# Attention: q and k turned by transposing transfers, sums folded and inverted in small form

## The chip, the cores and the metric

One core of one Trainium2 chip runs the whole program. The metric is the device time of one execution in microseconds (us); the runs of the kernel before lie between 1114.28 and 1118.21, with a median of 1114.59. Beside these runs one execution was taken by the hardware profiler. All rows come from it.

## The reference, cut to what matters

Three layers follow each other. The change is in the first.

```python
def rmsnorm(x, g):                       # q, k: (4, 12, 448, 64)
    return x / np.sqrt(np.mean(x * x, axis=-1, keepdims=True) + 1e-06) * g
q_n, k_n = rmsnorm(q, g_q), rmsnorm(k, g_k)
scores = 1.0 / np.sqrt(64) * np.matmul(q_n, k_n.transpose(0, 1, 3, 2))
attn = np.exp(scores - np.max(scores, axis=-1, keepdims=True))
attn = attn / (np.sum(attn, axis=-1, keepdims=True) + 1e-09)
x = np.matmul(attn, v)                   # rows: 4 * 448, columns: 12 * 64
# second layer: (sigmoid(x @ w_gate) * (x @ w_val)) @ w_out, 768 -> 1536 -> 768
# third layer: one of 8 experts per row, relu(x @ w1[e]) @ w2[e], 768 -> 1024 -> 768
```

## The kernel before

The 48 heads are worked on as 24 pairs (`PAIRS`); a pair is two heads of one batch, whose 64 columns stand side by side in 128. There are no queues worked out by a planner: the program of every engine is an order written by hand, and semaphores (`wait_ge`, `then_inc`) join them. The loop variable `n` of `STEPS` is a step. In step n TensorE computes the scores of pair n, weighs v with the probabilities of pair n-1 and computes the leading scores of pair n+1, from which the row maxima come.

The way of one pair through the engines:

- SP (SyncE) issues the load of q and k (`load_qk`, L457) as 112 rows with 4 x 64 x 2 numbers each for q and for k, and the loads of v (`load_v`, L463 and L468). It waits on nothing else in this part.
- ScalarE squares the rows (`take_squares`, L736), VectorE sums them per head (`mean_squares`, L979), GpSimd raises the means to the power -1/2 (`inverse_rms`, L566 and L569) and scales the rows of q and k in place (`normalise`, L578).
- TensorE turns the scaled rows by eight 112x128 transposes in f32 (`turn_qk`, L1389) into PSUM. ScalarE copies them as f16 (`high_qk`, L758 for q with the gain of both norms and L759 for k), VectorE writes what the f16 rounding left (`low_q` L1006, `low_k` L1013). Both halves are in `qk_t`, a ring of three.
- TensorE multiplies the high halves (`leading`, L1406, in four blocks j of 112 rows), VectorE takes the negated maxima (`maxima`, L1019), TensorE turns these (`turn_max`, L1413) and VectorE spreads them over the blocks (`shift_rows`, L1026).
- `scores(n, i)` (L1429, L1431), i from 0 to 3, are the full products in three f16 passes with the shift added. i = 0 holds the last 64 keys, the others 128 keys each. All four go to the same two banks of PSUM, so `scores(n, i+1)` waits for `exps(n, i)` on ScalarE (L765 for i = 0, L767 else).
- The probabilities of the last 64 keys are split in f16 halves (`end_high` L773 on ScalarE, `end_low` L606 on GpSimd), as is v (`v_high` L778, `v_low` L1033); TensorE weighs them in `weigh_end` (L1443). The 384 other keys are weighed in f32 (`weigh`, L1452), for each of the two heads h in three chunks; each product is two instructions. v stands beside a block of constants there, so the same product gives the row sums, 64 times the same.
- ScalarE copies the sums and the result to SBUF (`take_out(n, h)`, L785 and L786). VectorE inverts all 128x448 sums (`invert_sums`, L1039), GpSimd multiplies (`weigh_out`, L585), ScalarE and GpSimd split the result in two f16 halves (`x_high` L790, `x_low` L589) for the next layer.

What sets the order around the change: `weigh_end(n-1)` waits for `take_out(n-2, 1)`, because both use the same banks. `turn_qk` shares its banks with `leading`. ScalarE's program for one step is `take_out(n-2,1)`, `exps(n,0)`, squares, `end_high`, `exps(n,1)`, `take_out(n-1,0)`, `exps(n,2)`, `x_high`, `high_qk(n+2)`, `v_high`, `exps(n,3)`. Near the end it also splits the first weights of the second layer (`split_up`, L710, and `turned_high`, L716); on VectorE the corresponding part and the routing weights (L955, L967) wait for the last x. The first layer-two product (L1543) needs only the x of the first batch. L736 is also the line of the squares at the start, and L720 of the load of the constants, whose first 128 columns are the identity for the transposes. L1375 is filler work on TensorE at the start.

Of the kernel before, what the change touches and what calls it, by code (L numbers as in the profile page):

```python
# [18 lines left out]
S_OP = 256.0  # L19
# [38 lines left out]
def attention_moe_moe_kernel(nc, qk, v, v_last, g_qk, w_gate, w_val, w_out, w_out_t, router_w, out_gate_w,  # L58
# [14 lines left out]
    KCH = KEYS // 128  # L73
    assert S - KEYS == 64 == D
# [3 lines left out]
    with ctx:  # L78
# [55 lines left out]
        qk_t = [at.take(128, 4 * S, F16).rearrange("p (x l s) -> p x l s", x=2, l=2) for _ in range(3)]  # L134
# [6 lines left out]
        x_raw = [at2.take(128, S, F32) for _ in range(2)]  # L141
        sums = [at2.take(128, S, F32) for _ in range(2)]
# [113 lines left out]

        y_dram = nc.dram_tensor("y_parts", [N, 2 * DM], F16).ap()
# [3 lines left out]

        const_loaded = sem("const_loaded")
# [36 lines left out]
        sums_inv_ready = sem("sums_inv_ready")  # L299
# [141 lines left out]
        STEPS = range(PAIRS + 2)  # L441
# [4 lines left out]
        def _(sp):  # L446
# [7 lines left out]
            def load_qk(n):  # L454

                wait(sp, qk_turned, n - 3)
                sp.dma_start(qk_raw[n % 4].rearrange("p x j c -> p x (j c)"), qk_d[n]).then_inc(qk_loaded[n % 4], 16)  # L457
# [13 lines left out]
            load_qk(1)  # L471
            for n in range(2, 4):
                load_qk(n)
            for n in range(3):
                load_v(n)
            for n in range(4, PAIRS + 5):
                if 3 <= n - 5:
                    load_v(n - 5)
                if has(n):
                    load_qk(n)  # L480
# [80 lines left out]
        def _(pool):  # L561
            def inverse_rms(n):
# [3 lines left out]
                nc.gpsimd.tensor_scalar(rms_sq, mean_sq[n % 2], 1e-6, 1.0, ALU.add, ALU.mult).then_inc(rms_ready, 1)  # L566
                pool.wait_ge(rms_ready, n + 1)
# [3 lines left out]
            def normalise(n):  # L571

                pool.wait_ge(rms_inv_ready, n + 1)
                xs = slice(0, 1) if n == 0 else slice(0, 2)
# [6 lines left out]
            def weigh_out(n):  # L581

                pool.wait_ge(sums_inv_ready, n + 1)
                pool.wait_ge(o_taken, 4 * n + 4)
                nc.gpsimd.tensor_tensor(x_out[n % 2], x_raw[n % 2], sums_inv[n % 2], ALU.mult).then_inc(x_ready, 1)  # L585
# [24 lines left out]
            for n in STEPS:  # L610
# [3 lines left out]
                if has(n - 2):  # L614
                    weigh_out(n - 2)
                if has(n):
                    end_low(n)
                if has(n - 2):
                    x_low(n - 2)
# [85 lines left out]
        def _(act):  # L705
# [13 lines left out]
            act.dma_start(gains, g_qk).then_inc(gains_loaded, 16)  # L719
            act.dma_start(cst, consts).then_inc(const_loaded, 16)  # L720
# [39 lines left out]

            def exps(n, i):
# [18 lines left out]
            def take_out(n, h):  # L780

                act.wait_ge(o_ready, 2 * n + h + 1)
                wait(act, x_ready, n - 1)
                o_rows, sum_rows = slice(h * D, (h + 1) * D), slice((1 - h) * D, (2 - h) * D)
                nc.scalar.activation(sums[n % 2][o_rows], ps[sum_rows, 6 + h, SQ], ACT.Copy, bias=1e-9 * S_OP).then_inc(o_taken, 1)  # L785
                nc.scalar.activation(x_raw[n % 2][o_rows], ps[o_rows, 6 + h, SQ], ACT.Copy).then_inc(o_taken, 1)  # L786
# [19 lines left out]
            for n in STEPS:  # L806
                if n == 1:
                    load_up_weights()
                if n == 2:
                    load_router()  # L810
                if n == PAIRS - 3:
                    split_up(0, 0)
# [6 lines left out]
                if has(n + 4) and n > 0:  # L819
                    take_squares(n + 4 if n > 1 else 4)  # L820
                if has(n):
                    end_high(n)
                    exps(n, 1)
                if has(n - 1):
                    take_out(n - 1, 0)
                if has(n):
                    exps(n, 2)
                if n == 0:
                    exps(n, 3)
                if n == 1:  # L830
                    take_squares(5)
                if has(n - 2):
                    x_high(n - 2)
                if has(n + 2):
                    high_qk(n + 2)
                if has(n):
                    v_high(n)
                if has(n) and n > 0:
                    exps(n, 3)
# [102 lines left out]
        def _(dve):  # L942
# [93 lines left out]
            def invert_sums(n):  # L1036
                dve.wait_ge(o_taken, 4 * n + 3)
                wait(dve, x_ready, n - 1)
                nc.vector.reciprocal(sums_inv[n % 2], sums[n % 2]).then_inc(sums_inv_ready, 1)  # L1039
# [7 lines left out]
            dve.wait_ge(const_loaded, 16)  # L1047
# [10 lines left out]
            low_k(0)  # L1058
            shift_rows(0)
# [3 lines left out]
            for n in STEPS:  # L1063
                if has(n - 1):
                    v_low(n - 1)
                if has(n - 2):
                    invert_sums(n - 2)
                if has(n + 1):
                    maxima(n + 1, 0)
                    maxima(n + 1, 1)  # L1070
                if n == 1:
                    mean_squares(4)
                if has(n + 1):
                    maxima(n + 1, 2)
                    maxima(n + 1, 3)
                if has(n + 4) and n > 0:
                    mean_squares(n + 4)
                if has(n + 1):
                    shift_rows(n + 1)
                if has(n + 2):  # L1080
                    low_q(n + 2)
                    low_k(n + 2)
# [286 lines left out]
        def _(pe):  # L1369
# [24 lines left out]
            def leading(n, j):  # L1394

                if j == 0:
# [37 lines left out]
            def weigh_end(n):  # L1434

                pe.wait_ge(v_lo_ready, n + 1)
                pe.wait_ge(p_lo_ready, n + 1)
# [31 lines left out]
            pe.wait_ge(const_loaded, 16)  # L1469
# [24 lines left out]
            for n in STEPS[1:]:  # L1494
                if has(n):
                    scores(n, 0)
                if has(n + 1) and n > 1:
                    leading(n + 1, 0)
                if n == PAIRS:
# [229 lines left out]
```

## Time and profile before

| | |
|---|---|
| median of 3 runs | 1114.59 us |
| profiled execution: time / span | 1117.86 us / 1116.1 us |
| granted clock of TensorE, mean | 0.996 |
| busy over the span: TensorE products, VectorE, ScalarE, GpSimd | 98%, 53%, 38%, 22% |
| attention part, from the start to the first product of the second layer | 295.48 us |

The busy share is a mean over very different stages: in the attention part all engines are well used, in the later layers TensorE works nearly alone. So the attention part has to be read by itself, by stretches and by its timeline. The time of the profiled execution is 1.76 us longer than its span; the rows count from the span's start.

### The profile page before, as it was taken

The page shows a single profiled execution, that of the slowest core. Times are in us where ns is not written, and L with a number is a line of the kernel's source. Part 1 is how long each engine was busy: PE and PEld are TensorE (multiplying, and loading weights), DVE is VectorE, ACT ScalarE, POOL GpSimd, SP SyncE. Part 2 cuts the span into 40 slices and gives each one's busy share as a digit, 9 for nine tenths or more (in the row PEclk, how much of TensorE's full clock was granted, in tenths as well). Part 3 has the DMA queues.
Part 4 walks back from the last instruction along what each step waited for, and adds up shares of the span by engine and source line. Part 5 has one row for each costly group of instructions (what it writes and reads, how often), then busy time and mean ns, then how long its engine had stood idle before and what let it go on. Part 6 is the DMA issues. An engine that isn't in the chain of part 4 may idle for free.

```text
span 1116.1 us, 17825 instructions
## 1 busy us (share of the span) xinstructions
PE 1092.4 (98%) x6616; PEld 571.7 (51%) x6617; DVE 594.7 (53%) x840; ACT 428.6 (38%) x632; POOL 250.0 (22%) x237
## 2 busy tenths in 40 slices
PE   7999999999999999999999999999999999999997
PEld 3444444443455555555555555556455555555554
DVE  6889888887633333333343331104565555556841
ACT  5777787777511111111111220001343443443531
POOL 4767676772200000000000100000111112111211
PEclk9999999999999999999999999999999999999999
DMA  5522121200121111111100332100375455456710
GB/s 137 135 52 73 51 74 51 71 22 18 43 86 57 58 56 56 56 56 56 56 29 1 119 136 70 43 28 29 138 252 190 156 185 204 142 194 225 270 36 18
DMA packets 72026, 104.11 MB, mean 93 GB/s; under 512 B 29344, under 2 KB 47918, under 8 KB 71968
## 3 DMA queue, kind: packets, MB, share of 16 engines
q1 hardware_dynamic: 63536, 89.84, 24.7%
q0 software_dynamic: 3168, 11.02, 2.9%
q10 hardware_dynamic: 5264, 2.49, 0.9%
q8 instruction: 36, 0.59, 0.2%
q14 instruction: 22, 0.18, 0.1%
HBM read 93.88 MB, written 13.76 MB: 96 GB/s over the span
## 4 chain that ended last, share of the span: by engine, by line
PE 93%; DMA 2%; ACT 2%; DVE 1%; issue 1%; ACTq 0%; POOL 0%; POOLq 0%; DVEq 0%; SPq 0%
PE ps L1543 29%; PE ps L1558 14%; PE ps L1615 12%; PE ps L1637 12%; PE ps L1452 10%; PE ps L1429 5%; PE ps L1406 2%; PE ps L1389 2%; PE ps L1443 2%; PE ps L1431 1%; PE ps L1624 1%; PE ps L1602 1%; DMA arena<-y_parts,arena 1%; DMA arena<-in_constants 1%; PE ps L1684 1%
## 5 line engine op out<-in xcount | busy, mean ns | idle before, releaser
L1543 PE MATMUL ps<-arena 128*128 128x448 f16 x1728 | 328.8, 352 | 0.0
L1543 PEld LDWEIGHTS ps<-arena 128*128 128x128 f16 x1728 | 168.2, 98 | 156.1 <-issue 0.5
L1558 PE MATMUL ps<-arena 128*128 128x392 f16 (+1 forms) x996 | 165.3, 329 | 0.0
L1615 PE MATMUL ps<-arena 128*128 128x512 f16 x648 | 147.3, 382 | 1.2 <-DVE arena L1322 1.2
L1123 DVE SCALAR_TENSOR_TENSOR arena<-arena 128x768 f16<-128x768 f32 (+1 forms) x112 | 112.8, 1068 | 65.3 <-ACT arena L878 64.5
L1637 PE MATMUL ps<-arena 128*128 128x384 f16 x816 | 135.4, 326 | 0.0
L1452 PE MATMUL ps<-arena 128*128 128x448 f32 x288 | 132.2, 569 | 0.0
L1558 PEld LDWEIGHTS ps<-arena 128*128 (+1 forms) x996 | 97.3, 98 | 66.9
L845 ACT ACTIVATE arena<-ps 128x448 f32<-128x448 f32 x48 | 26.1, 544 | 262.7 <-PE ps L1543 262.6
L1097 DVE SCALAR_TENSOR_TENSOR arena<-ps,arena 128x448 f32<-128x448 f32 x48 | 30.0, 625 | 175.6 <-PE ps L1543 95.7
L878 ACT ACTIVATE arena<-arena 128x768 f16<-128x768 f32 (+1 forms) x112 | 99.3, 928 | 41.6 <-DMA arena<-in_moe_w 37.4
L1019 DVE TENSOR_REDUCE arena<-ps 112x2 f16<-112x896 f32 x96 | 99.0, 1077 | 17.1 <-PE ps L1406 17.1
L1637 PEld LDWEIGHTS ps<-arena 128*128 128x128 f16 x816 | 79.1, 98 | 50.6
L1615 PEld LDWEIGHTS ps<-arena 128*128 128x128 f16 x648 | 62.9, 98 | 73.1 <-issue 2.4
L767 ACT ACTIVATE arena<-ps,arena 128x896 f32<-128x896 f32 x72 | 72.5, 1008 | 27.7 <-PE ps L1431 27.6
L1039 DVE RECIPROCAL arena<-arena 128x448 f32<-128x448 f32 x24 | 70.9, 2953 | 10.4 <-ACT arena L785 10.4
L660 POOL MEMSET arena<- 128x1536 f16 x1 | 1.4, 1378 | 323.8 <-PE ps L1543 323.8
L1429 PE MATMUL ps<-arena 64*128 64x448 f16 (+1 forms) x576 | 71.1, 352 | 1.9 <-DVE arena L1026 0.7
L1452 PEld LDWEIGHTS ps<-arena 128*128 128x128 f32 x288 | 47.4, 190 | 45.3 <-issue 45.3
L1157 DVE TENSOR_SCALAR arena<-ps 128x16 f32 (+1 forms) x12 | 2.1, 175 | 112.4 <-ACT arena L862 112.4
L569 POOL TENSOR_TENSOR arena<-arena 112x16 f32<-112x16 f32 x21 | 60.9, 2901 | 1.8
L862 ACT ACTIVATE arena<-ps 128x768 f16<-128x768 f32 x13 | 10.5, 811 | 126.3 <-PE ps L1558 126.3
(181 smaller groups left out, 1045.5 us busy)
## 6 DMA issues: line engine op xcount, KB each, us to landing
arena<-in_moe_w SPq DMA_DIRECT2D x48, 512.0 KB, 4.8
arena<-in_moe_w SPq DMA_DIRECT2D x64, 384.0 KB, 4.7
arena<-in_qk SPq DMA_DIRECT2D x23, 448.0 KB, 3.6
y_parts<-arena SPq DMA_DIRECT2D x16, 384.0 KB, 2.3
arena<-in_v SPq DMA_DIRECT2D x48, 96.0 KB, 2.5
arena<-in_moe_w_out SPq DMA_DIRECT2D x12, 384.0 KB, 5.3
arena<-in_w_out_t SPq DMA_DIRECT2D x11, 384.0 KB, 3.1
arena<-in_moe_w_gate SPq DMA_DIRECT2D x10, 384.0 KB, 4.2
```

Of the source, the lines that this page charges most:

```text
L569: nc.gpsimd.tensor_tensor(rms_inv, rms_sq, minus_half, ALU.pow).then_inc(rms_inv_ready, 1)
L767: nc.scalar.activation(probs[n % 2][:, :, i - 1], ps_pair(score_slot(n, i), 128), ACT.Exp, bias=lift[:, 1:2])\
L878: nc.scalar.activation(hi, raw_rows(e, p), ACT.Copy, scale=S_OP).then_inc(w_hi_ready, 1)
L1019: nc.vector.tensor_reduce(neg_max[n % 2][:, :, j], ps_pair(max_slot(n, j)), AX_X, ALU.max, negate=True)\
L1039: nc.vector.reciprocal(sums_inv[n % 2], sums[n % 2]).then_inc(sums_inv_ready, 1)
L1123: nc.vector.scalar_tensor_tensor(lo, raw_rows(e, p), S_OP, hi, ALU.mult, ALU.subtract).then_inc(w_lo_ready, 1)
L1429: nc.tensor.matmul(outs[h], qk_t[n % 3][rows, 1, kl, ks], qk_t[n % 3][rows, 0, ql], start=(kl + ql == 0), stop=False)
L1452: last = nc.tensor.matmul(ps[:, 6 + h, SQ], v_ones[n % 3][:, c, h * D:h * D + 2 * D], probs[n % 2][:, h, c], start=False, stop=(c == KCH - 1))
L1543: last = nc.tensor.matmul(ps[:, 2 * (b % 2) + g, 0:S], up_w[s][:, g, c, wl], xt[:, b * KC + c, xl], start=(c == 0 and wl + xl == 0), stop= ...
L1558: last = nc.tensor.matmul(ps[:, 4 + 2 * s + h, 0:cols], gt[:, f, gl, bass.ds(t * 128, 128)], wo[:, f, wl, h, 0:cols], start=(f == 0 and gl ...
L1615: last = nc.tensor.matmul(ps[:, b, :], x_t[:, xl, c], w1_s[s][:, c, wl, b * 512:(b + 1) * 512], start=(c == 0 and xl + wl == 0), stop=(c = ...
L1637: last = nc.tensor.matmul(ps[:, 4 + h, 0:HALF_DM], hid_t[:, b, hl, c], w2_s[s][k][:, wl, h * HALF_DM:(h + 1) * HALF_DM], start=(k == 0 and ...
```

## The change

1. From pair 5 on (`TURNED = 5`, the sixth) TensorE does not turn q and k. GpSimd multiplies the rows of q by both gains (`gain_rows`, prepared once by VectorE from a new input `g_rows`) before it scales; ScalarE writes the f16 copy of the rows (`rows_high`), VectorE the rest (`rows_low`), and SP issues two transposing transfers, one for each f16 half, from the rows to `qk_t`, whose layout is changed for it. `leading(n, 0)` waits for them.
2. The sums are not inverted 128x448 wide. SP moves one row of each head's sums into 64 partitions of 7 (`move_sums`), VectorE inverts 128x7, SP saves the result in HBM, waits for this, and loads it spread over 64 partitions again (`spread_inverse`). `weigh_out`, `x_high` and `x_low` come one step later, so `STEPS` has one more; `x_raw` and `sums` have three buffers.
3. `end_low` goes from GpSimd to VectorE from the fourth pair on, and from step 3 on the orders of TensorE, ScalarE and VectorE are written anew. Steps 0 to 2 keep the old order nearly.
4. The constants are loaded in two pieces, the identity first (`eye_loaded`); the gains' load goes from ScalarE's queue to SP's.

```diff
-        STEPS = range(PAIRS + 2)
+        STEPS = range(PAIRS + 3)
...
+            def move_sums(n):
+                sp.wait_ge(o_taken, 4 * n + 3)
+                wait(sp, few_inv_ready, n - 1)
+                for h in range(2):
+                    sp.dma_start(few_sums[n % 2][h * D:(h + 1) * D],
+                                 sums[n % 3][h * D:h * D + 1].rearrange("o (p c) -> o p c", c=S // D)).then_inc(sums_moved[n % 2], 16)
+            def move_rows(n):
+                sp.wait_ge(rows_lo_ready, n - TURNED + 1)
+                sp.wait_ge(scores_ready, 4 * (n - 2))
+                for l in range(2):
+                    sp.dma_start_transpose(qk_t_blocks[n % 3][:, l], rows_parts[n % 2][:, l]).then_inc(qk_moved[n % 3], 16)
+            def spread_inverse(n):
+                sp.wait_ge(few_inv_ready, n + 1)
+                wait(sp, x_ready, n - 1)
+                sp.dma_start(inv_dram[n % 2].rearrange("h (p c) -> (h p) c", c=S // D), few_inv[n % 2]).then_inc(inv_saved[n % 2], 16)
+                sp.wait_ge(inv_saved[n % 2], 16 * (n // 2) + 16)
+                for h in range(2):
+                    sp.dma_start(sums_inv[n % 2][h * D:(h + 1) * D], inv_dram[n % 2, h].unsqueeze(0).to_broadcast([D, S]))\
+                        .then_inc(inv_spread[n % 2], 16)
+            for n in range(2, PAIRS + 2):
+                move_sums(n - 2)
+                if has(n + 1):
+                    load_v(n + 1)
+                if n + 2 >= TURNED and has(n + 2):
+                    move_rows(n + 2)
+                if has(n + 6):
+                    load_qk(n + 6)
+                spread_inverse(n - 2)
...  GpSimd, in inverse_rms(n)
+                if n >= TURNED:
+                    pool.wait_ge(gain_rows_ready, 1)
+                    nc.gpsimd.tensor_tensor(qk_raw[n % 4][:, 0], qk_raw[n % 4][:, 0], gain_rows.unsqueeze(1).to_broadcast([PT, J, 2 * D]),
+                                            ALU.mult).then_inc(q_gained, 1)
...  GpSimd, loop of the steps: x one step later
-                if has(n - 2):
-                    weigh_out(n - 2)
-                if has(n):
+                if has(n - 3):
+                    weigh_out(n - 3)
+                    x_low(n - 3)
+                if n < 3:
                     end_low(n)
...  ScalarE
-            act.dma_start(gains, g_qk).then_inc(gains_loaded, 16)
-            act.dma_start(cst, consts).then_inc(const_loaded, 16)
+            act.dma_start(cst[:, 0:128], consts[:, 0:128]).then_inc(eye_loaded, 16)
+            act.dma_start(cst[:, 128:CONST_COLS], consts[:, 128:CONST_COLS]).then_inc(const_loaded, 16)
...
+            def rows_high(n):
+                act.wait_ge(qk_normed, n + 1)
+                if n - 2 >= TURNED:
+                    act.wait_ge(qk_moved[(n - 2) % 3], moved(n - 2))
+                nc.scalar.activation(rows_parts[n % 2][:, 0], qk_raw[n % 4].rearrange("p x j c -> p (x j c)"), ACT.Copy)\
+                    .then_inc(rows_hi_ready, 1)
...  ScalarE's steps from 3 on
                     take_out(n - 2, 1)
                     exps(n, 0)
+                    end_high(n)
+                    v_high(n)
+                    exps(n, 1)
+                    take_squares(n + 4)
+                    exps(n, 2)
+                x_high(n - 3)
                     take_out(n - 1, 0)
                     exps(n, 3)
+                    rows_high(n + 3)
...  VectorE
             def invert_sums(n):
-                nc.vector.reciprocal(sums_inv[n % 2], sums[n % 2]).then_inc(sums_inv_ready, 1)
+                dve.wait_ge(sums_moved[n % 2], 32 * (n // 2) + 32)
+                nc.vector.reciprocal(few_inv[n % 2], few_sums[n % 2]).then_inc(few_inv_ready, 1)
...  VectorE's steps from 3 on: rows_low(n+2), maxima(n+1,0), v_low(n), maxima(n+1,1), end_low(n),
...  invert_sums(n-2), maxima(n+1,2), mean_squares(n+4), maxima(n+1,3), shift_rows(n+1)
...  TensorE's steps from 3 on
                     scores(n, 0)
                     leading(n + 1, 0)
+                    leading(n + 1, 1)
                     weigh_end(n - 1)
-                    weigh(n - 1, 0, (0,))
-                    leading(n + 1, 1)
                     scores(n, 1)
-                    weigh(n - 1, 0, (1, 2))
+                    weigh(n - 1, 0, (0,))
                     leading(n + 1, 2)
-                    leading(n + 1, 3)
+                    weigh(n - 1, 0, (1,))
                     scores(n, 2)
+                    weigh(n - 1, 0, (2,))
+                    leading(n + 1, 3)
                     weigh(n - 1, 1, (0,))
-                    turn_qk(n + 2)
                     scores(n, 3)
                     turn_max(n + 1)
                     weigh(n - 1, 1, (1, 2))
```

## Rows read from the trace of the kernel before

**Rows 1.** Busy time of each engine in one stretch of the attention part.

```profile
core 0: us, PE busy (x) PEld busy (x) DVE busy (x) ACT busy (x) POOL busy (x), PEclk, DMA share, GB/s
...
140.00:160.00 20.00, 19.84 (x118) 8.25 (x116) 17.69 (x18) 15.42 (x25) 15.36 (x12) 1.00 0.25 70
```

**Rows 2.** TensorE's timeline over one step: start, duration, line.

```profile
153.01 0.76 PE L1429 MATMUL ps<-arena 64*64 64x448 f16 x6
...
153.88 0.40 PE L1406 MATMUL ps<-arena 64*112 64x448 f16 x2
154.36 0.74 PE L1443 MATMUL ps<-arena 64*128 64x448 f16 x6
155.03 1.02 PE L1452 MATMUL ps<-arena 128*128 128x448 f32 x2
155.98 0.40 PE L1406 MATMUL ps<-arena 64*112 64x448 f16 x2
156.22 0.73 PE L1429 MATMUL ps<-arena 64*128 64x448 f16 x6
...
157.06 1.77 PE L1452 MATMUL ps<-arena 128*128 128x448 f32 x4
158.77 0.59 PE L1406 MATMUL ps<-arena 64*112 64x448 f16 x4
...
160.04 1.02 PE L1452 MATMUL ps<-arena 128*128 128x448 f32 x2
...
161.76 0.74 PE L1429 MATMUL ps<-arena 64*128 64x448 f16 x6
...
164.34 0.76 PE L1429 MATMUL ps<-arena 64*64 64x448 f16 x6
```

**Rows 3.** ScalarE's timeline in the same step.

```profile
153.12 0.54 ACT L785 ACTIVATE arena<-ps 64x448 f32<-64x448 f32 x1 [0.42 <-PE ps L1452]
...
154.77 1.05 ACT L736 ACTIVATE arena<-arena 112x1024 f32<-112x1024 f32 x1
155.72 0.57 ACT L773 ACTIVATE arena<-arena 128x448 f16<-128x448 f32 x1
157.18 1.01 ACT L767 ACTIVATE arena<-ps,arena 128x896 f32<-128x896 f32 x1 [0.89 <-PE ps L1431]
```

**Rows 4.** VectorE's groups by shape, first 345 us: count | busy us, mean ns.

```profile
L1039 DVE RECIPROCAL arena<-arena 128x448 f32<-128x448 f32 x24 | 70.9, 2953 | 10.4 <-ACT arena L785 10.4
...
L1103 DVE TENSOR_TENSOR arena<-arena 128x448 f16<-128x448 f32 x7 | 4.4, 626 | 0.2
```

**Rows 5.** Timeline of the start, ScalarE's queue and three engines.

```profile
1.27 0.45 ACTq L719 DMA_DIRECT2D arena<-in_g_qk  x1
...
7.00 1.47 POOL L578 TENSOR_TENSOR arena<-arena 112x512 f32<-112x512 f32 x1 [4.69 <-DVE arena L993]
...
9.81 1.06 ACT L736 ACTIVATE arena<-arena 112x1024 f32<-112x1024 f32 x1 [1.95 <-DMA arena<-in_qk]
...
10.46 1.13 PE L1389 MATMUL ps<-arena 112*128 112x112 f32 x8 [3.27 <-DMA arena<-in_constants]
```

**Rows 6.** The SP queue's issues in one step, with their time.

```profile
139.19 0.32 SPq L457 DMA_DIRECT2D arena<-in_qk  x1
141.78 1.24 SPq L463 DMA_DIRECT2D arena<-in_v  x2
```

**Rows 7.** DMA from 100 to 200 us: size of one, us to landing.

```profile
arena<-in_qk SPq DMA_DIRECT2D x9, 448.0 KB, 3.5
...
arena<-in_v_last SPq DMA_DIRECT2D x17, 16.0 KB, 2.4
```

**Rows 8.** DMA of the first 12 us, the gains' load.

```profile
arena<-in_g_qk ACTq DMA_DIRECT2D x1, 1.0 KB, 5.8
```

**Rows 9.** Timeline of the last steps and the hand-over.

```profile
257.32 0.74 PE L1443 MATMUL ps<-arena 64*128 64x448 f16 x6 [1.06 <-ACT arena L786]
...
302.00 0.19 DVE L967 TENSOR_SCALAR arena<-ps 128x32 f32<-128x32 f32 x1 [2.96 <-POOL arena L589]
```

**Rows 10.** The chain that ended last, start and length.

```profile
295.48 23.84 PE ps L1543 x126
```

More of the change, by code:

```diff
@@ L73, in attention_moe_moe_kernel @@
     KCH = KEYS // 128
+    TURNED = 5
     assert S - KEYS == 64 == D
@@ L805, in _ @@
             high_qk(1)
-            for n in STEPS:
+            for n in range(3):
                 if n == 1:
@@ L810, in _ @@
                     load_router()
+                    take_out(0, 1)
+                exps(n, 0)
+                if n > 0:
+                    take_squares(n + 4 if n > 1 else 4)
+                end_high(n)
+                exps(n, 1)
+                if n > 0:
+                    take_out(n - 1, 0)
+                exps(n, 2)
+                if n == 0:
+                    exps(n, 3)
+                if n == 1:
+                    take_squares(5)
+                high_qk(n + 2)
+                v_high(n)
+                if n > 0:
+                    exps(n, 3)
+            rows_high(TURNED)
+            for n in STEPS[3:]:
                 if n == PAIRS - 3:
@@ L826, in _ @@
                 if has(n):
-                    exps(n, 2)
-                if n == 0:
                     exps(n, 3)
[L830 to L839, printed above, removed]
+                if has(n + 3):
+                    rows_high(n + 3)
             def chunk(f, s):
@@ L1062, in _ @@
             mean_squares(3)
-            for n in STEPS:
-                if has(n - 1):
+            for n in range(3):
+                if n > 0:
                     v_low(n - 1)
+                maxima(n + 1, 0)
+                maxima(n + 1, 1)
+                if n == 1:
+                    mean_squares(4)
+                if n == 2:
+                    dve.wait_ge(gain_rows_loaded, 16)
+                    nc.vector.scalar_tensor_tensor(gain_rows, gain_raw[:, 0:2 * D], float(D) ** -0.5, gain_raw[:, 2 * D:4 * D],
+                                                   ALU.mult, ALU.mult).then_inc(gain_rows_ready, 1)
+                    invert_sums(0)
+                maxima(n + 1, 2)
+                maxima(n + 1, 3)
+                if n > 0:
+                    mean_squares(n + 4)
+                shift_rows(n + 1)
+                low_q(n + 2)
+                low_k(n + 2)
+            v_low(2)
+            for n in STEPS[3:]:
+                if has(n + 2):
+                    rows_low(n + 2)
+                if has(n + 1):
+                    maxima(n + 1, 0)
+                if has(n):
+                    v_low(n)
+                if has(n + 1):
+                    maxima(n + 1, 1)
+                if has(n):
+                    end_low(n)
                 if has(n - 2):
@@ L1068, in _ @@
                 if has(n + 1):
[L1069 to L1073, printed above, removed]
                     maxima(n + 1, 2)
[L1075 to L1076 removed]
+                if has(n + 4):
                     mean_squares(n + 4)
                 if has(n + 1):
+                    maxima(n + 1, 3)
                     shift_rows(n + 1)
[L1080 to L1082 removed]
                 if n == PAIRS - 2:
@@ L1493, in _ @@
             turn_max(1)
-            for n in STEPS[1:]:
+            for n in range(1, 3):
+                scores(n, 0)
+                if n > 1:
+                    leading(n + 1, 0)
+                weigh_end(n - 1)
+                weigh(n - 1, 0, (0,))
+                if n == 1:
+                    leading(n + 1, 0)
+                leading(n + 1, 1)
+                scores(n, 1)
+                weigh(n - 1, 0, (1, 2))
+                leading(n + 1, 2)
+                leading(n + 1, 3)
+                scores(n, 2)
+                weigh(n - 1, 1, (0,))
+                turn_qk(n + 2)
+                scores(n, 3)
+                turn_max(n + 1)
+                weigh(n - 1, 1, (1, 2))
+            for n in STEPS[3:]:
                 if has(n):
                     scores(n, 0)
-                if has(n + 1) and n > 1:
+                if has(n + 1):
                     leading(n + 1, 0)
+                    leading(n + 1, 1)
                 if n == PAIRS:
```

106 lines of the change are left out of this document (73 added, 33 removed).

## The prediction

> **What bounds the kernel now.** I read the table of stretches first. In a stretch in the middle of the attention part TensorE is busy 19.84 of 20 us at full granted clock; VectorE is next with 17.69, then ScalarE with 15.42 and GpSimd with 15.36 [rows 1]. So here TensorE is the bound. Its timeline then gives the period: pair by pair the same order repeats, from the first `scores` product at 153.01 to the next at 164.34, 11.33 us [rows 2]. The reader should take the starts, not the busy times, because matmuls overlap. The chain of waits says the same thing. From the moment TensorE starts on the next layer the change touches nothing. What moves the time is therefore the attention stage: start, 24 steps, hand-over.
>
> **Steady steps (3 to 20, 18 of them).** Removed: the eight `turn_qk` transposes. Two f32 products of `weigh`, the turn behind them and the start of `scores` take 160.04 to 161.76, 1.72; two such products with an f16 product right behind take 155.03 to 155.98, 0.95 [rows 2]. The turn is worth 0.77 us.
>
> Moved: `leading(n+1,1)` now stands ahead of `weigh_end`. In the old order TensorE has one `leading` between `scores` and `weigh_end`, starting at 153.88, and `weigh_end` starts 0.48 later; one `leading` elsewhere needs 0.24 (155.98 to 156.22) [rows 2]. The missing 0.24 is a wait: `weigh_end` needs both copies of `take_out`, which ScalarE began at 153.12, and starts 1.24 after that [rows 2, 3]. The second `leading` fills exactly this hole: 0.24 saved.
>
> Added: the f32 products of `weigh` stand in five groups, not four. Four products at once take 1.71 (157.06 to 158.77), two take 0.95, so the split costs 2 x 0.95 - 1.71 = 0.19 [rows 2]. TensorE alone: 11.33 - 0.77 - 0.24 + 0.19 = 10.51.
>
> ScalarE now has `rows_high` between the last exponentials and `take_out`. The square of 112x1024, 1.05 long, starts 0.95 before its successor [rows 3], so I take 0.95 for the copy of the same shape and 0.91 for exponentials of 1.01 by the same overlap. The last `scores` starts 2.58 before the next step [rows 2]; exponentials start 0.96 after their `scores` (157.18 against 156.22) [rows 2, 3]. So they start at -1.62, `rows_high` at -0.71, `take_out` at +0.24 instead of +0.11. `weigh_end` may then start at 0.24 + 1.24 = 1.48, and TensorE is there at 0.87 + 2 x 0.24 = 1.35. A wait of 0.13 remains: 10.64 a step. Saving 18 x 0.69 = 12.4. Bounds: 14.8 if there is no such wait; 7.9 if `rows_high` and the exponentials cost their full durations and the wait is 0.38.
>
> The other engines: VectorE has 17.69 of 20, which is 10.0 a step [rows 1]. It loses the 2.95 us reciprocal, gains `rows_low` (no row of this shape; at least the 0.63 of a 448-wide subtraction, at most 1024/448 of it, 1.43; I take 1.4) and `end_low` at 0.63 [rows 4]. That is 9.1 with `low_q` and `low_k` still counted, below 10.64. The small reciprocal is 1/64 as wide; I cost it at 0.2. GpSimd has 8.7, gains the q gain (the 512-wide multiplication took 1.47 [rows 5]) and loses a subtraction of about 1.0: 9.2, hidden by the 10.64 of TensorE. ScalarE has 8.7, gains 0.95, loses the two copies of `high_qk`: hidden except for the 0.13 above. If this cover were gone, VectorE or GpSimd would have to be 1.5 us slower a step to count.
>
> **The SP queue** is the dangerous term, because everything there is in one row and blocks. A step issues: two `move_sums`, four loads of v, two transposing transfers, one load of q and k, one save, a wait for that save, two spreads. Issue times: 1.24 for two loads of v, so 0.62 each, which I take for every transfer of short pieces, and 0.32 for the load with long rows [rows 6]. `move_sums` 1.24, v 2.50, qk 0.32, save to landing 2.4 like the 16 KB load [rows 7], spreads 0.64 to 1.24: 7.1 to 7.7, I take 7.4. With T for one transposing issue the queue's loop is 7.4 + 2T. It stays hidden under 10.64 up to T = 1.62. No row shows T. Nearest from below 0.32, from above 0.62 [rows 6]; if each of a transfer's eight 112x128 blocks cost such an issue, T would be 8 x 0.62 = 5.0. I take a value between 0.6 and 1.6, nearest to the rows of one issue, and cost it at nothing, hidden by TensorE's step. The transfers carry 229 KB each; the 448 KB load lands in 3.5 [rows 7], so both together should land in about 4. They are issued at about 4.6 into the step (`take_out`'s first copy at 0.8, `move_sums` and v 3.74) and are needed at 0.87 of the next: 6.9 us of room. The Trainium skill, in "DMA: Bandwidth & Descriptors", section "Latency and other measured facts", gives 261 GB/s for a DMA transpose; an estimate from it is 458 KB / 261 GB/s = 1.8 us for both, and the sum would stay as it is. No row of this trace shows a transposing transfer, so nothing here confirms it.
>
> The sums' way is hidden: folded sums are wanted by VectorE after `end_low`, about 5.2 into the step, and land at 0.8 + 0.6 + 2.4 = 3.8. If they were late by more than 1.4, the third and fourth `maxima` and then `turn_max` would be next.
>
> **Start.** TensorE's first turn begins at 10.46, released by the constants' DMA [rows 5]. It needs only the identity, now a load of its own in the place of the gains' one, which was issued at 1.27 and landed 5.8 later, at 7.1 [rows 5, 8]. The scaled q was ready at 7.00 + 1.47 = 8.47, so at most 1.9 is gained. But ScalarE squares pair 2 at 9.81, for 1.06, ahead of the first `high_qk` [rows 5], which can pull the gain to 0.9 or, if the loads land otherwise, to 0. I take -1.5.
>
> **Entry into step 3.** GpSimd's gain for pair 5 waits for VectorE's `gain_rows`, which stands behind two maxima in step 2; the scaling and `rows_high(5)` follow, and `take_out` stands behind that. I take +0.5, from 0 to 1.5.
>
> **Steps 21 to 23.** In step 21 `weigh_end` waited 1.06 for ScalarE's split of weights [rows 9]; that split stays, so nearly nothing comes back. Step 22 loses its wait and gets the order's gain, 0.6; step 23 merges its weigh groups, 0.5. Together -1.2.
>
> **Hand-over.** VectorE got the last x at 302.00 after a wait of 2.96 on GpSimd, 6.5 after TensorE began the next layer at 295.48 [rows 9, 10]. Now three transfers of about 2.4 replace the 2.95 reciprocal [rows 4, 7]: some 5 later, 11.5 to 12 after that start. TensorE waits for the first gate result only after four sums of 18 products, and 126 products take 23.84 there [rows 10], so after 13.6. Up to 2 us of cover, of which ScalarE's gate itself takes about half. I take +0.5, from 0 to 3.
>
> **Sum:** -12.4 - 1.5 + 0.5 - 1.2 + 0.5 = -14.1. The profiled execution took 1117.86 (span 1116.1, 1.8 around it), so it becomes 1103.8; it lies 3.3 above the median of 1114.59. On the median: 1100.5.
>
> **Rivals.** (a) As forecast, 1097 to 1105: 0.50.
> (b) The SP queue sets the step mildly, T between 1.62 and 1.9, or ScalarE's wait is the full 0.38: the step is 10.9 to 11.2 and the time 1105 to 1111. For it speaks that the queue is within 1.6 us of the step at T = 0.8; against it that an ordinary issue takes 0.32 to 0.62. 0.20.
> (c) Slower: the transposing issue holds SP for T over 2.0. From there the loop, 7.4 + 2T, passes 11.33 by more than start and end give back. At T = 2.5 it is 12.4, 19 x 1.07 = +20, less the 1.7 of start and end: 1133. For it: a wait for a landing and a dozen issues share one queue which before was idle most of a step; save and spreads stand behind 458 KB and the next 448 KB load. 0.22 with (d).
> (d) The transfers run block by block, each block its own fixed cost. With the row of 0.62 per block, 16 blocks are 9.9 and the loop is 17.3: 19 x 6.0 = +114, 1226. This part of (c) has 0.07. A page of the Trainium skill, "VectorE: DVE Perf Modes", section "The three transpose paths", speaks this way: 1309 ns for one 128x128 by DMA against 390 by TensorE. Taken block after block its figure would be an estimate of 21 us a pair; nothing in this trace bears it out.
> (e) No change: gains and a slightly long queue cancel, T near 1.96, 1109 to 1120: 0.08.
>
> A measurement of this kernel can tell about 0.5%, 5.6 us, from no change. Faster by more: (a) and most of (b), 0.65. Within: the rest of (b) and (e), 0.12. Slower: 0.23. The range runs from 1097 (no ScalarE wait and the full start: -14.8 - 1.9 - 1.2) to 1128, T = 2.4; (d) and the upper part of (c), about 0.15, are left out. The likeliest case alone has 1097 to 1105.
>
> **What would show it.** Right: the period from `scores(n,0)` to the next at 10.6 to 10.8; `leading(n+1,0)` released by TensorE's own order, not by a DMA; SP idle at the top of `move_sums`; `weigh_end` waiting about 0.1 on `take_out`; TensorE's first turn at about 8.6. Wrong: `leading` with a wait on a DMA, transposing issues over 1.7 us, SP's wait for `o_taken` gone, VectorE waiting for the sums.

## The result

The changed kernel took 1126.94 us (median, 1124.74 to 1127.79) against 1116.07 for the kernel before (four runs each): ratio 1.0096, 95% interval 1.008 to 1.0113. It is slower by about 11 us, where 14 less were forecast. It lies inside the stated range, among the slower outcomes, to which 0.23 was given.

The stretch of the attention part that answers to [rows 1], with its columns in the same order (TensorE, its weight loads, VectorE, ScalarE, GpSimd):

```profile
140.00:160.00 20.00, 17.07 (x96) 6.08 (x94) 14.85 (x17) 14.83 (x22) 14.85 (x11) 1.00 0.51 126
```

No engine is near 20 of 20 (TensorE has 17.07), at full granted clock. No engine that computes is the bound. TensorE's timeline over one step, against [rows 2]:

```profile
146.24 0.76 PE L1551 MATMUL ps<-arena 64*64 64x448 f16 x6
...
154.34 0.74 PE L1551 MATMUL ps<-arena 64*128 64x448 f16 x6
154.92 0.35 PE L1553 MATMUL ps<-arena 64*128 64x448 f16 x2
156.41 0.22 PE L1535 MATMUL ps<-arena 112*128 112x112 f16 x1 [1.14 <-DVE arena L1104]
156.47 1.73 PE L1577 MATMUL ps<-arena 128*128 128x448 f32 x4
158.13 0.76 PE L1551 MATMUL ps<-arena 64*64 64x448 f16 x6
```

This step is 158.13 - 146.24 = 11.89. Read the same way, steps 3 to 20 vary from 10.7 to 13.9 and have a mean of 12.16 where they had 11.33. The hole is before `turn_max` (L1535), which waits for the last `maxima` (L1104) on VectorE. The waits of all engines from 60 to 240 us (engine, line, released by: us in total, times, longest) say what VectorE waited for:

```profile
PEld ps L1535 <- DVE arena L1104: 25.4, 14, 2.7
...
DVE arena L1125 <- DMA arena<-arena: 21.0, 13, 2.4
```

L1125 is the small reciprocal. It waits for `move_sums`, and behind it stand two `maxima` and the squares' sums. So the sums are late. SP's own waits in the same window have only two rows, and neither is the wait for `take_out` at the top of `move_sums`:

```profile
SPq L530 <- DMA sums_inv<-arena: 49.6, 15, 3.8
SPq L490 <- PE ps L1577: 1.1, 2, 0.6
```

L530 is the first spread, which waits for the save of the inverses to land. L490, a load of v that waits for its buffer, is the only other wait, 1.1 us in all; otherwise SP is always issuing or waiting for the save. Its timeline over one round, to set beside [rows 6], and the landings, beside [rows 7]:

```profile
138.69 1.18 SPq L513 DMA_DIRECT2D arena<-arena  x2
139.91 1.26 SPq L490 DMA_DIRECT2D arena<-in_v  x2
141.22 1.26 SPq L495 DMA_DIRECT2D arena<-in_v_last  x2
142.57 2.60 SPq L521 DMA_TRANSPOSE arena<-arena  x2
145.22 0.58 SPq L484 DMA_DIRECT2D arena<-in_qk  x1
145.91 0.36 SPq L527 DMA_DIRECT2D sums_inv<-arena  x1
149.35 1.10 SPq L530 DMA_DIRECT2D arena<-sums_inv  x2
150.55 1.18 SPq L513 DMA_DIRECT2D arena<-arena  x2
```

```profile
arena<-in_qk SPq DMA_DIRECT2D x8, 448.0 KB, 4.2
...
arena<-arena SPq DMA_TRANSPOSE x16, 2.7
sums_inv<-arena SPq DMA_DIRECT2D x8, 3.5 KB, 3.6
```

One round is 150.55 - 138.69 = 11.86, of which 3.44 pass between the start of the save (145.91) and the spreads (149.35). A save of 3.5 KB lands after 3.6 us. The load of q and k of 448 KB and both transposing transfers were issued just ahead of it. The Trainium skill, "DMA: Bandwidth & Descriptors", section "Queues, rings and completion order", says that each DMA engine takes the descriptors of a ring in order and that the semaphore's increment lands only after every earlier write of that engine. By that rule the small save pays for the 448 KB. The trace agrees: the load lands after 4.2 (median), at 145.22 + 4.2 = 149.4, and the save at 145.91 + 3.6 = 149.5.

The same trace has the save with only one of the two kinds of traffic ahead of it. In the round before the first transposing transfer the load of q and k stands ahead alone: the save starts at 47.26 and the spreads at 50.49, 3.23 later. In the first round that has no load of q and k left, the transposing transfers stand ahead alone: 244.21 to 245.84, 1.63.

**The clock.** Once in this part TensorE's granted clock fell to half, the lower of its two levels (1.2 instead of 2.4 GHz), from 232.1 to 235.5, behind an idle time of 2.11 us:

```profile
231.47 0.22 PE L1535 MATMUL ps<-arena 112*128 112x112 f16 x1 [2.11 <-DVE arena L1104]
231.53 2.75 PE L1577 MATMUL ps<-arena 128*128 128x448 f32 x4
234.20 1.33 PE L1551 MATMUL ps<-arena 64*64 64x448 f16 x6
```

Four f32 products took 2.75 where they took 1.73 in the step above. The longest step, 13.87, is this one; from the four products to the next `leading` it lost 1.64. No stretch of the kernel before has this from 20 to 320 us. That is at most 1.6 of the 11 us here.

### The profile page after: what moved, and what is told of

The parts are those of the page before. It is cut to its first block, busy times and chain, and to the rows that moved or that the text cites. A ratio compares the mean times of both kernels' runs of the same rounds, so it can differ in the third digit from the quotient of the medians.

```text
span 1126.0 us, 17723 instructions
## 1 busy us (share of the span) xinstructions
PE 1082.2 (96%) x6464; PEld 552.7 (49%) x6465; DVE 560.7 (50%) x843; ACT 430.5 (38%) x613; POOL 254.7 (23%) x235
## 4 chain that ended last, share of the span: by engine, by line
PE 78%; SPq 9%; DMA 6%; DVE 2%; issue 2%; ACT 1%; ACTq 0%; POOL 0%; POOLq 0%; DVEq 0%
PE ps L1684 29%; PE ps L1699 15%; PE ps L1778 12%; PE ps L1756 12%; DMA sums_inv<-arena 5%; PE ps L1577 4%; SPq L521 3%; PE ps L1551 2%; SPq L490 1%; PE ps L1765 1%; SPq L530 1%; SPq L513 1%; SPq L495 1%; PE ps L1743 1%; DVE arena L1104 1%
## 5 line engine op out<-in xcount | busy, mean ns | idle before, releaser
L1577 PE MATMUL ps<-arena 128*128 128x448 f32 x288 | 138.3, 580 | 0.0
L1104 DVE TENSOR_REDUCE arena<-ps 112x2 f16<-112x896 f32 x96 | 103.1, 1082 | 25.4 <-PE ps L1528 25.4
L1551 PEld LDWEIGHTS ps<-arena 64*128 64x128 f16 (+1 forms) x576 | 22.3, 97 | 60.4 <-issue 41.7
```

The costliest lines, as they stand in the source:

```text
L1104: nc.vector.tensor_reduce(neg_max[n % 2][:, :, j], ps_pair(max_slot(n, j)), AX_X, ALU.max, negate=True)\
L1551: nc.tensor.matmul(outs[h], qk_t[n % 3][rows, 1, kl, ks], qk_t[n % 3][rows, 0, ql], start=(kl + ql == 0), stop=False)
L1577: last = nc.tensor.matmul(ps[:, 6 + h, SQ], v_ones[n % 3][:, c, h * D:h * D + 2 * D], probs[n % 2][:, h, c], start=False, stop=(c == KCH - 1))
```

## The experiments

Theory A: SP's in-order queue sets the step, through its wait for a save that lands late. Rivals: B, the transposing transfers are themselves late and `leading` waits for them; C, the new order or a slowed VectorE (`v_low` takes longer, see the end) sets the step; D, the sums' way through memory is too long by itself. The times of before in the three comparisons were 1115.98, 1115.95 and 1115.87.

**Save first.** Only SP's order changes; all the work stays.

```diff
                 move_sums(n - 2)
                 load_v(n + 1)
+                save_inverse(n - 2)
                 move_rows(n + 2)
-                load_qk(n + 6)
-                spread_inverse(n - 2)      # save, wait, spread
+                spread_inverse(n - 2)      # wait, spread
+                load_qk(n + 6)
```

> All work of the changed kernel stays; on SP's queue the save of the inverses now stands ahead of the two transposing transfers, the wait for it and the spreads behind them, and the load of q and k last. Theory A (SP's queue sets the step, by its in-order wait of 3.4 to 4.2 us for the save, which landed behind 448 KB of q and k and the transposing transfers): the queue's work falls to 1.20 + 1.22 + 2.65 + 0.4 + 2.65 + 0.69 = 8.8 us plus at most 0.5 of wait, below TensorE's own step, so steps go from a mean of 12.1 to 10.6 to 10.9 and the time from 1127 to about 1100. Rival B (the transposing transfers are late in themselves): leading still waits for them, the step stays above 11.3, time above 1115. Rival C (the new order, with v_low of 1.36 us instead of 0.28 on VectorE, sets the step): the step stays above 11.3 with turn_max waiting for VectorE, time above 1115.

Measured: 1107.63, ratio to before 0.9925 (0.9909 to 0.9942), and 19 us under the changed kernel. The save's landing (transfers from 100 to 200 us) and SP's waits (60 to 240 us) in this kernel:

```profile
sums_inv<-arena SPq DMA_DIRECT2D x10, 3.5 KB, 1.4
```

```profile
SPq L527 <- DVE arena L1129: 17.6, 16, 1.4
SPq L513 <- ACT arena L862: 13.7, 17, 2.7
```

SP no longer waits for the save's landing. It waits for VectorE's small reciprocal ahead of the save (L527), and it is idle at the top of `move_sums` (L513), as the prediction had said it should be. Most steps are 10.93 to 10.95, and the mean over steps 3 to 20 is 11.01: 18 x (12.16 - 11.01) = 20.7, slightly more than the 19.3 by which the time fell. The layers behind the attention part differ by up to 3 us between traces (818.0 to 820.8) without relation to the change, so the two agree. A holds and B and C fall. The saving was expected at 27 and is 19: the mean step is 11.01 and not some 10.75, which is 4.7 us over 18 steps, and the expected 27 was more than 18 steps from 12.1 to 10.75 give, 24.

**The q and k load last.** Only `load_qk(n + 6)` moves behind `spread_inverse(n - 2)`; the transposing transfers are still ahead of the save.

> All work stays; only the load of q and k moves behind the spreads on SP's queue, so the save no longer stands behind its 448 KB. Theory A in its form 'the q and k load ahead in the rings makes the save late': the save lands in about 2.4 instead of 3.6, the loop shortens by about 1.3 to 10.8, the step is 10.8 to 11.0, time about 1104. Theory A in its other form (the transposing transfers ahead of the save, not the load, delay it): the save still needs 3 us or more, loop about 12, time 1120 or more. Rivals B and C: no change, 1125 to 1128.

Measured: 1108.60, ratio 0.9939 (0.9923 to 0.9956). The save's landing here, from 100 to 200 us (1.4 in the kernel with the save first):

```profile
sums_inv<-arena SPq DMA_DIRECT2D x9, 3.5 KB, 1.6
```

So what made the save late is the load of 448 KB, 2.0 of the 3.6 us; the transposing transfers ahead of it make 0.2. They carry as many bytes, but the first is issued some 2.7 us ahead of the save and lands after 2.7. Moving one line of the program gives 18 of the 19 us.

**No save, no spreads.** The inverse is computed but neither saved nor spread; the result is multiplied by a constant, so the division by the sums is left out.

```diff
-                spread_inverse(n - 2)
...
-                pool.wait_ge(inv_spread[n % 2], 32 * (n // 2) + 32)
+                pool.wait_ge(few_inv_ready, n + 1)
```

> The inverses are computed but neither saved nor spread; the result is multiplied by a constant, so the division by the sums is left out. Turning by transfers, all orders and the folding of the sums stay. Theory A: the queue's work is 1.22 + 2.65 + 2.65 + 0.69 = 7.2 us, nothing waits on it; the step is that of TensorE with the new order, 10.6 to 10.9; time about 1099, the same as with the save first within 3 us. Rivals B and C: steps above 11.3, time above 1115.

Measured: 1106.22, ratio 0.9917 (0.9901 to 0.9934). Steps are 10.93 to 10.95, mean 11.01, as in the kernel with the save first. So in that kernel, with all its transfers, the queue costs nothing more. The level itself is 7 us above what was expected.

**The sums alone.** The kernel before with `move_sums`, the small reciprocal, save and spreads, x one step later; TensorE still turns every pair. The load of q and k stands behind the spreads here, so the save has no large load ahead of it.

> The kernel before with the sums' part of the change alone: folded, inverted 128x7, saved and spread by transfers, x one step later, q and k loaded behind the spreads. TensorE turns all pairs, all other orders are those of before. Theory A: the queue's work is 1.20 + 1.22 + 2.65 + 0.36 + 2.4 + 0.5 = 8.3 us, under TensorE's 11.33, so each part by itself is hidden: time within 3 us of before, 1113 to 1118. Rival D (the sums' way through memory is too long in itself, whatever else is queued): steps longer than 11.33, time above 1120.

Measured: 1116.72, ratio 1.0007 (0.9997 to 1.0016). Every step is 11.33, as before, and the save lands after 1.6. D falls. Whether the save behind the load would have been hidden in this kernel was not run. The 2.95 us that VectorE no longer spends are worth nothing, as TensorE is the bound there.

**One transfer more.** The changed kernel with one more load a step.

```diff
                 move_sums(n - 2)
+                wait(sp, spare_loaded, 16 * (n - 2))
+                sp.dma_start(spare, v_last[n - 2, 0:D]).then_inc(spare_loaded, 16)
```

> The changed kernel with one more transfer a step on SP's queue (16 KB of v into an unused place, issue 0.60 to 0.65). Theory A: SP's queue sets the step, so all of it shows: 0.65 x 20 steps = 13, 1140. If other waits share the bound, less. Rivals B and C (the queue is not the bound): no change, 1125 to 1129.

Measured: 1136.30, ratio 1.0192 (1.0175 to 1.0209), 9.4 more than the changed kernel. The mean step went from 12.16 to 12.65, by 0.49. The issue took 0.59, and the next one began 0.64 after it (155.28 to 155.92). The queue's own rounds, from one `move_sums` to the next while q and k are still loaded (16 rounds), went from a mean of 12.43 to 12.97, by 0.54. SP's waits from 60 to 240 us show that it waited for nothing but the save here too, a little shorter (3.24 a round against 3.31):

```profile
SPq L532 <- DMA sums_inv<-arena: 45.4, 14, 3.5
SPq L492 <- PE ps L1582: 0.6, 3, 0.2
```

So nearly all of an added issue shows, as A says. TensorE's granted clock fell to half five times in this trace, some 20 us in all, which makes single steps as long as 15.5; the queue waited only 0.6 us for TensorE, so its rounds don't come from that.

**Grouped products, on the kernel with the save first.**

```diff
                     scores(n, 1)
-                    weigh(n - 1, 0, (0,))
+                    weigh(n - 1, 0, (0, 1))
                     leading(n + 1, 2)
-                    weigh(n - 1, 0, (1,))
                     scores(n, 2)
-                    weigh(n - 1, 0, (2,))
                     leading(n + 1, 3)
+                    weigh(n - 1, 0, (2,))
                     weigh(n - 1, 1, (0,))
...  VectorE
-                    mean_squares(n + 4)
                     maxima(n + 1, 3)
+                    mean_squares(n + 4)
```

> On the kernel with the save first, TensorE's order from step 3 on groups the f32 products: after scores 1 four at once, then leading 2, scores 2, leading 3, four at once; VectorE takes the squares' sums behind the last maxima. With the save first a step was 10.94, of which a leading before f32 products took 0.33 and two f32 products with f16 behind 0.95. Theory E (each change between f16 and f32 products costs TensorE, 0.19 on the way back and 0.09 on the way in, and the new order has two more than needed): two groups fewer and one end of another save about 0.56, step 10.4, minus 11 over 20 steps: about 1097. Rival F (the step is set by ScalarE's chain, last scores, exponentials, rows_high, take_out, weigh_end): the step stays at 10.8 or more with weigh_end waiting for take_out, time above 1105.

Measured: 1096.32, ratio 0.9823 (0.9803 to 0.9843), 11.3 under the kernel with the save first. Most steps are 10.30, the mean is 10.51. TensorE in the ungrouped kernel with the save first, and then in this one:

```profile
152.07 1.02 PE L1581 MATMUL ps<-arena 128*128 128x448 f32 x2
153.02 0.40 PE L1532 MATMUL ps<-arena 64*112 64x448 f16 x2
153.35 1.02 PE L1581 MATMUL ps<-arena 128*128 128x448 f32 x2
154.30 0.74 PE L1555 MATMUL ps<-arena 64*128 64x448 f16 x6
```

```profile
157.29 1.77 PE L1582 MATMUL ps<-arena 128*128 128x448 f32 x4
158.99 0.40 PE L1533 MATMUL ps<-arena 64*112 64x448 f16 x2
159.22 0.73 PE L1556 MATMUL ps<-arena 64*128 64x448 f16 x6
```

The same four f32 products and one `leading` take 152.07 to 154.30, 2.23, in the first and 157.29 to 159.22, 1.93, in the second. A `leading` with f32 products behind it takes 0.33, one with f16 behind 0.23. Two such places a step, 0.30 each, are 0.60 of the 0.64 by which the common step fell. E holds; F (the chain over ScalarE sets the step) falls.

**Grouped products, on the changed kernel.** The same edit with SP's queue left as it was.

> The changed kernel with TensorE's and VectorE's grouped order alone, SP's queue as in the changed kernel. With the save first this order was worth 11 us. Theory A: the queue sets the step, so a shorter order of TensorE is worth nothing while it does: 1124 to 1128. If order and queue added up, 1116.

Measured: 1124.80, ratio 1.0077 (1.0048 to 1.0106), 2.1 under the changed kernel, with intervals that overlap; the 1116 of a sum of both lies outside. The edit that is worth 11 us when TensorE is the bound is worth about 2 here, not told from nothing. The queue's rounds have a mean of 12.50, against 12.43. Behind them, where the queue no longer counts, step 22 is 10.09 in place of 10.73, but step 21 is 13.78 where the grouped kernel has 11.67: the granted clock fell to half there, from 270.4 to 273.8. Without that the edit might show 2 us more (an estimate, 13.78 - 11.67).

**Transposing transfers of four blocks.** On the kernel with the save first, each of the two transfers is cut in two of four 112x128 blocks.

> On the kernel with the save first each transposing transfer is cut in two of four 112x128 blocks, so four issues a step. If the issue holds the queue in proportion to the blocks (1.28 for eight, so 0.65 for four), the queue's work is unchanged and the step stays 10.94. If 1.28 is mainly a fixed cost, four issues are 5.1, the queue's work passes 11.3 and the step goes to 11.3 or more, time above 1113.

One execution was taken, without a comparison: 1134.14. The issues of the transposing transfers in the kernel with eight blocks and in this one (count: shortest, median, longest ns):

```profile
L521 SPq DMA_TRANSPOSE arena<-arena x38: 1242/1282/1362, 55.0 to 256.4; - x38
```

```profile
L522 SPq DMA_TRANSPOSE arena<-arena x76: 1190/1255/2364, 55.0 to 284.7; - x76
```

Half the blocks take the queue as long as all of them, so four issues add 2.5 to its round. The mean step is 12.40. More than the queue's own round is in that: from 60 to 240 us `leading` waited 16.1 us for the transposing transfers and SP 10.7 us for VectorE's small reciprocal, so a late transfer came back to the queue through TensorE and VectorE.

**One transposing transfer.** The changed kernel with both halves in one transfer of sixteen blocks.

```diff
-            return 32 * ((n - TURNED) // 3 + 1)
+            return 16 * ((n - TURNED) // 3 + 1)
...
-                for l in range(2):
-                    sp.dma_start_transpose(qk_t_blocks[n % 3][:, l], rows_parts[n % 2][:, l]).then_inc(qk_moved[n % 3], 16)
+                sp.dma_start_transpose(qk_t_blocks[n % 3].rearrange("p l b m -> p (l b) m"),
+                                       rows_parts[n % 2].rearrange("p l c -> p (l c)")).then_inc(qk_moved[n % 3], 16)
```

> The changed kernel with its two transposing transfers of eight 112x128 blocks joined to one of sixteen, the queue's order as in the changed kernel. A transfer of four blocks held SP's queue 1.26 us, one of eight 1.28. Theory G (the issue of a transposing transfer costs the queue a fixed 1.25 or so): the queue's loop falls by 1.3, from 12.2 to 10.9, just under the 10.94 of the new order; time between 1106 and 1112. Rival H (above eight blocks the issue grows with the blocks): 2.6 for one, the time stays at 1125 to 1128.

Measured: 1113.45, ratio 0.9978 (0.9969 to 0.9988). One issue now takes

```profile
L520 SPq DMA_TRANSPOSE arena<-arena x19: 1345/1514/1763, 54.6 to 259.3; - x19
```

and the mean step is 11.34. It is much nearer to G than to H, though not all of G: the issue takes 1.26 to 1.28 up to eight blocks and 0.23 more with sixteen, and the time is 1.5 over the 1106 to 1112 that G gave. The queue's work falls by 2 x 1.28 - 1.51 = 1.05 a round, which gives back 13 us; with the save still behind 448 KB (it landed after 3.8) the queue stays the bound in part of the steps.

**Both.** The grouped kernel with the joined transfer.

> The kernel with the save first and the f32 products grouped, with the two transposing transfers joined. Under theory A the queue no longer sets the step there (10.30 in most steps, 10.4 to 10.8 in some), so a shorter queue brings nothing but perhaps those few: within 3 us of the grouped kernel's 1096, at best 1093. If the queue still sets some of it, the mean step falls from 10.51 to 10.30, 4 us.

Measured: 1095.84, ratio 0.9817 (0.9801 to 0.9834). With the grouped kernel's 1096.32 the intervals overlap. The shorter queue brings nothing that can be measured once it is not the bound. These two are the fastest versions, 20 us under the kernel before.

**The identity first, on the kernel before.**

```diff
-            act.dma_start(gains, g_qk).then_inc(gains_loaded, 16)
-            act.dma_start(cst, consts).then_inc(const_loaded, 16)
+            act.dma_start(cst[:, 0:128], consts[:, 0:128]).then_inc(eye_loaded, 16)
+            act.dma_start(cst[:, 128:CONST_COLS], consts[:, 128:CONST_COLS]).then_inc(const_loaded, 16)
...  SP, behind load_qk(1)
+            sp.dma_start(gains, g_qk).then_inc(gains_loaded, 16)
```

> The kernel before with its constants loaded in two pieces, the identity first, and the gains on SP's queue. As forecast, the first turn comes at 8.4 instead of 10.5, but the first exponential's way behind the squares of pair 2 lets 1.5 of it through: the first scores at about 18.4 instead of 19.9, time 1.5 lower than before, 1114.5, which the rounds can hardly tell. Rival: the gain is given back by the loads of the first weights on ScalarE's queue in step 1, then the scores of step 3 start at 51.0 as before.

Measured: 1114.69, ratio 0.9991 (0.998 to 1.0002), which is not told from no change, as expected. In the trace the first scores are at 16.95 against 19.91 and those of step 3 at 48.09 against 51.03, so nothing is given back by step 3. But this point moves by itself: the first scores are at 18.21 in the changed kernel and at 17.03 in the one with one transfer more, though both start alike, and at 19.36 in the kernel with the sums alone, which starts like the kernel before. In the traces the start comes 1.2 to 3.0 us earlier; in the runs of this kernel 1.3 of it shows, and that is not told from nothing.

## Why the prediction was wrong, point by point

The step that failed is the price of SP's queue, "7.1 to 7.7, I take 7.4" beside 2T, and with it the claim that the queue stays hidden behind TensorE. T itself was right: 1.28, inside "a value between 0.6 and 1.6". With 7.4 and 1.28 the loop would have been 10.0 and hidden. The round of the timeline above is 11.86, less 2.65 for the transposing transfers, so 9.21: 1.8 more than taken. By the rows from 138.69 to 150.55:

- Save and wait: 3.44, taken at 2.4 "like the 16 KB load". This is the largest part, 1.04 of the 1.8. The prediction named the traffic ahead of the save in rival (c) and gave it no price. With the load of 448 KB elsewhere the save lands after 1.4 to 1.6, so the row of the 16 KB load was even too dear for it; what was missing was the queue ahead of it.
- Load of q and k: 0.69, where 0.32 was taken, as when it is issued alone.
- The spreads 1.20, at the upper end of the 0.64 to 1.24 that was given.
- v and its ends 2.66, the folded sums 1.22: 0.1 more than taken, gaps.

What follows from the late loop went as the prediction stated it for that case: SP's idle time at `move_sums` is gone, VectorE waits for the folded sums, and "the third and fourth `maxima` and then `turn_max` would be next". Rival (c) was right in place and sign, but it asked for T over 2.0; at T = 1.28 the part beside 2T decided it. That T fell inside the forecast is partly luck: no row showed it, and it is twice the row of one issue that was held nearest. Apart from one wait of 1.6 `leading` did not wait for the transposing transfers, which landed after 2.7.

**Steady steps.** The forecast of 10.64 can be held against the kernel with the save first: 10.94. The turn's 0.77 and the wait of `weigh_end` went as stated. The split of the f32 products was priced at 0.19 for the way back to f16 only; the way from `leading` into f32 products costs another 0.09, twice a step. The last `scores` to `turn_max` is 0.94 for 0.86, a small wait for VectorE. `weigh_end` starts 1.52 after `scores` (149.12 to 150.64), for 1.48. These make up the 0.30. Steps 3 and 4 are 11.74 and 11.40 in that kernel (step 3 is 11.7 to 11.8 in all with the new order): entry costs 1.3 where +0.5 was taken. Together 18 x (11.01 - 10.64) = 6.7, of which the forecast had 0.5 as entry. That covers the 5.7 by which this kernel's saving, 8.4 against its own comparison, falls short of the forecast 14.1.

**Start.** -1.5 was taken. The traces show 1.2 to 3.0, the runs 1.3, as said above. The first turn was at 8.40, for the 8.6 forecast.

**End.** Step 21 is 12.31 as before in the kernel with the save first, steps 22 and 23 gain. Its last scores to the second layer are 286.94 - 270.53 = 16.4, against 17.05 before: the longer way of the last sums is hidden, the +0.5 was not needed.

**Slips in the working.** The bound of 7.9 is too low: full durations add 0.10 for `rows_high` and 0.10 for the exponentials, so the wait is 0.33, not 0.38, and the bound 8.8. The three transfers at the hand-over, less the reciprocal, are 3 x 2.4 - 2.95 = 4.3, not 5. The two transposing transfers together carry as many bytes as the load of 448 KB. None of these moves the outcome.

## What to carry to other kernels

A wait for a small transfer costs what its queue has in flight ahead of it: price it with the traffic ahead, not by the row of a similar transfer issued alone (a load of 448 KB just ahead cost 2.0 us here; other sizes were not tried), and issue a small transfer that somebody waits for before the large one that nobody waits for. Whether the save would also have been late on another queue beside the same load was not tried. When work leaves a saturated engine for a queue that also blocks, add up the queue's whole round, issues and landings, against the step. The prediction did so with a landing priced too low; the same work was hidden as soon as the order was right. And as long as another resource sets the step, a better order of the former bottleneck shows next to nothing; it had its 11 us once the queue was mended.

## What the runs showed of the hardware

A transposing transfer held SP's queue 1.26 us with four 112x128 blocks, 1.28 with eight and 1.51 with sixteen; most other issues there take 0.32 to 0.62. It landed after 2.4, 2.7 and 3.6.

A save of 3.5 KB landed after 1.4 us with nothing large just ahead of it in its queue, after 1.6 behind two transposing transfers, and after 3.6 to 3.8 behind a load of 448 KB.

From 20 to 320 us TensorE's granted clock fell to half only in the four traces in which TensorE was least busy: once in the changed kernel (TensorE busy 271 of these 300 us), five times with one transfer more (269), three times with the transposing transfers of four blocks (267) and with the grouped products alone (262). The kernel before (292 of 300) and all the others kept the full clock, the one with the joined transfer (284) too.

VectorE's `v_low`, 128x128, took 0.32 in the mean before and 1.0 in the changed kernel. The kernel with the save first shows it beside GpSimd's scaling, and at another time beside the raising to a power:

```profile
151.49 1.90 POOL L648 TENSOR_TENSOR arena<-arena 112x1024 f32<-112x1024 f32 x1
152.00 1.54 DVE L1122 SCALAR_TENSOR_TENSOR arena<-arena 128x128 f16<-128x128 f32 x1 [0.36 <-ACT arena L855]
```

```profile
52.31 2.90 POOL L638 TENSOR_TENSOR arena<-arena 112x16 f32<-112x16 f32 x1
52.58 0.29 DVE L1122 SCALAR_TENSOR_TENSOR arena<-arena 128x128 f16<-128x128 f32 x1 [0.36 <-ACT arena L855]
```

In the first it ends at 153.54, just behind GpSimd's instruction (153.39). The Trainium skill, "SBUF — State Buffer", section "SBUF: two separate sides", has VectorE with two inputs from SBUF and GpSimd lock each other out for a whole instruction; the first pair of rows agrees, the second does not show it. No experiment took this wait away, so that it costs any of the step is not shown.
